# Long convolution and two mixture-of-experts layers: tokens packed without padding columns, and a new order of work in three places

## The chip, the cores and the metric

The kernel runs on one core of a Trainium2 chip. The metric is the time of one execution on the device in microseconds; the median of several executions counts.

## The reference, cut to what matters

```python
# attn: x, v [2, 11456, 128]; pos_emb [11456, 64]; w1 [64, 64]; w2 [64, 128]
h_filt = (np.maximum(pos_emb @ w1, 0.0) @ w2) * np.exp(-0.01 * pos)[:, None]
Uf = np.fft.rfft(x * v, n=2 * S, axis=1)
Hf = np.fft.rfft(h_filt, n=2 * S, axis=0)
x = x * np.fft.irfft(Uf * Hf[None], n=2 * S, axis=1)[:, :S, :]      # then [22912, 128]
# twice (the first time with modality_bias[modality_id] added to the logits):
logits = x @ w_gate                                   # 8 experts
e_idx = argmax(logits); gate_w = softmax(logits)[e_idx]
for e in range(8):
    out[mask] = gate_w[mask, None] * (np.maximum(x[mask] @ w1[e], 0.0) @ w2[e])   # w1 [128, 1024]
```

All matrices are fp32. A long causal convolution per channel is followed by two layers in which each token goes to one of eight experts.

## The kernel before, in words

There are four stages, each a block of its own with a barrier of all engines behind it: the convolution up to its inner inverse (`convolution`), the outer inverse with the first routing (`inverse_stage`), and two expert stages (`experts`, called with `then` for the first, which also routes for the second).

**Convolution.** The sequence is laid out as a two-dimensional transform: J = 91 columns (held as JP = 96) by 128 samples, 181 outer frequencies of which 92 are kept (K1), 128 inner ones. It begins with the filter. In 16 groups TensorE makes the hidden layer (`hidden`, L288), VectorE applies ReLU and window (L458) into one of two buffers `weighed`, TensorE makes four outputs of 2 x 128 columns (`output`, L295), and ScalarE copies the group with two activations, even and odd (L393), into `stage`. When all are copied ScalarE issues four stores of the filter's upper 64 channels to memory (`h_d`, L398); SP's signal loads (`load_signals`, L217) wait for these stores, since they go to the same slots. Then for each half of the channels (half 0, half 1):

- *Transform.* 24 chunks in the order `ORDER`: F chunks are of the filter, S chunks of signals (x times v). TensorE makes eight matmuls a chunk (L311) into one of two PSUM halves; ScalarE (L364 to L369) and VectorE (F chunks only, L425, L427) evict them into `A`. VectorE's `mix` multiplies x and v (L415) and folds them (L419), `LEAD[half]` chunks ahead of the chunk that uses them. LEAD is 2 in the first half and 3 in the second.
- *Spectral loop.* T = 46 steps. `forward(t)` on TensorE (L321, two matmuls of 384 columns), `filter_out(t)` on ScalarE (L376), `multiply(t)` on VectorE (L434, two operations), `combine(t)` on VectorE (L445, L447), `inverse(t)` on TensorE (L330, two of 256 columns), `back_out(t)` on ScalarE (L383), store by SP. TensorE's order is forward(t), inverse(t-2); VectorE's is multiply(t), combine(t-1). SP loads each step's matrices six steps ahead.

**Inverse stage.** TensorE begins with six warm-up matmuls on `inv`, for whose load it waits (L822). In 16 groups: `outer` (L793, 32 matmuls of 96 columns a half), ScalarE's copy (L929), VectorE's `mix` (L847 into `y`, L853 into `x1T`), `gate` (L808) on six chunks of 128 tokens a group, ScalarE's copies (L940, L943), VectorE's `choose` and `put`, which give each token its row among those of its expert (the last operations of a group are L887 and L888), and 12 scatters on POOL (L1000), one for each 128 tokens. Columns 91 to 95 are padding and are routed to nowhere. After group i's scatters POOL waits for those of group i - 1 in `settle`. VectorE ends the stage with `finish`, which copies the experts' end rows to `ends_i` (L666) and computes the table of tiles (up to L699); then SP writes a block of padding rows behind each expert (`Router.pad`, L709) and waits for them.

**Expert stages.** 49 tiles of 512 tokens in a software pipeline (`pipeline`); each engine runs its steps with a lag in tiles. L1162 to L1164 are the first layer, L1179 to L1181 the second, L1263 scales the results into `rows[s]` (four buffers), POOL scatters them (four a tile, L1381 or L1385). POOL's list of steps is `[(settle, 1), (scatter, 0)]`: before tile k it waits for the scatters of tile k - 1. ScalarE's scaling of tile k waits for `rows_free`, that is for settle(k - 4), in the first expert stage; in the second VectorE's `meta` does. The first expert stage ends with `finish` and `pad` as well. L1366 is POOL's first operation of an expert stage.

## Time and profile before

| | us |
|---|---|
| runs | 2048.15, 2060.18, 2061.36 |
| median | 2060.18 |
| profiled execution | 2052.0 |
| its span | 2050.2 |
| TensorE busy in the span | 1843.9 (90%) |
| VectorE, ScalarE, GpSimd busy | 1242.7, 1001.2, 583.7 |

Stages on the axis of the span: filter phase to 47.9, transforms and spectral loops to about 450, inverse stage to 752, first expert stage to 1424, second to 2050.2. A row of the timeline has the start, the duration, the engine, the line of the kernel, the operation with its tiles and shapes, how many instructions are merged, and in brackets how long the engine was idle before and what ended that. A fp32 matmul has two records. A queue's name (ACTq, SPq) marks the issue of a DMA, not the transfer.

### The profile page before, as it was taken

How to read it: one execution, taken by the hardware profiler on the slowest of the kernel's cores; microseconds unless marked ns; L12 is line 12 of the kernel's file. 1: busy time of each engine (PE TensorE's matmuls, PEld its weight loads, DVE VectorE, ACT ScalarE, POOL GpSimd, SP SyncE). 2: the span in 40 equal slices, each digit the busy share in tenths (PEclk: the TensorE clock that was granted, in tenths of full speed). 3: DMA queues.
4: the chain of work that ended last, by engine and by line, in shares of the span. 5: the costliest groups of instructions: out<-in, count | busy, mean ns of one | idle time of the engine just before them, and what ended most of it. 6: DMA issues, size and time to landing. Idle time of an engine off the chain costs nothing. (4 is left out here: it accounts for less than half of the span.)

```text
span 2050.2 us, 34634 instructions
## 1 busy us (share of the span) xinstructions
PE 1843.9 (90%) x9508; PEld 1547.3 (75%) x9508; DVE 1242.7 (61%) x3396; ACT 1001.2 (49%) x2185; POOL 583.7 (28%) x603
## 2 busy tenths in 40 slices
PE   8789988989989619999999999993999999999986
PEld 6665576559989517888888888893788888888886
DVE  1668776754767716777777777764555555555542
ACT  3563376432333305555555555551555555555543
POOL 0000000002777750333333333334033333333323
PEclk9899999987888759999999999996999999999998
DMA  4858694767999747777777777683666665665682
GB/s 142 218 140 254 202 235 141 214 186 216 323 301 319 241 155 272 239 250 255 250 253 252 247 252 254 242 326 119 245 232 207 225 234 207 225 234 207 229 308 110
DMA packets 193268, 469.51 MB, mean 229 GB/s; under 512 B 24691, under 2 KB 75455, under 8 KB 192792
## 3 DMA queue, kind: packets, MB, share of 16 engines
q1 hardware_dynamic: 163288, 412.13, 61.2%
q0 software_dynamic: 18688, 35.99, 4.9%
q10 hardware_dynamic: 11200, 20.26, 2.9%
q8 instruction: 45, 0.74, 0.2%
q14 instruction: 47, 0.39, 0.1%
HBM read 366.14 MB, written 105.28 MB: 230 GB/s over the span
## 5 line engine op out<-in xcount | busy, mean ns | idle before, releaser
L1306 DVE SCALAR_TENSOR_TENSOR m_hid<-m_pH,m_hid 128x512 fp32r<-128x512 f32 x784 | 540.9, 690 | 449.8 <-ACT m_hid L1241 443.9
L1241 ACT ACTIVATE m_hid<-m_pH 128x512 fp32r<-128x512 f32 x784 | 470.5, 600 | 534.4 <-PE m_pH L1164 534.4
L1162 PE MATMUL m_pH<-m_xT,m_w 128*128 128x512 f32 (+1 forms) x864 | 347.5, 402 | 7.8 <-DMA m_w<-halves 5.2
L1179 PE MATMUL m_pO<-m_hid,m_w 128*128 128x512 f32 (+1 forms) x864 | 323.0, 374 | 10.3 <-issue 10.3
L1381 POOL DMA_INDIRECT rows<-m_rows,m_idx x196 | 190.5, 972 | 476.9 <-ACT m_rows L1263 415.0
L1164 PE MATMUL m_pH<-m_xT,m_w 128*128 128x512 f32 (+1 forms) x864 | 323.3, 374 | 0.0
L1163 PE MATMUL m_pH<-m_xT,m_w 128*128 128x512 f32 (+1 forms) x864 | 322.5, 373 | 0.0
L1181 PE MATMUL m_pO<-m_hid,m_w 128*128 128x512 f32 (+1 forms) x864 | 321.5, 372 | 0.0
L1180 PE MATMUL m_pO<-m_hid,m_w 128*128 128x512 f32 (+1 forms) x864 | 320.3, 371 | 0.0
L1385 POOL DMA_INDIRECT out_dram<-m_rows,m_token x196 | 190.4, 972 | 429.8 <-ACT m_rows L1263 367.9
L1000 POOL DMA_INDIRECT rows<-oi_rows,oi_idx x192 | 196.4, 1023 | 102.0 <-issue 92.7
L1179 PEld LDWEIGHTS m_pO<-m_hid,m_w 128*128 128x128 f32 x864 | 163.9, 190 | 40.0 <-issue 11.5
L1162 PEld LDWEIGHTS m_pH<-m_xT,m_w 128*128 128x128 f32 x864 | 164.9, 191 | 28.6 <-DMA m_w<-halves 5.9
L1164 PEld LDWEIGHTS m_pH<-m_xT,m_w 128*128 128x128 f32 x864 | 164.0, 190 | 29.6
L1181 PEld LDWEIGHTS m_pO<-m_hid,m_w 128*128 128x128 f32 x864 | 163.8, 190 | 29.6
L1180 PEld LDWEIGHTS m_pO<-m_hid,m_w 128*128 128x128 f32 x864 | 164.0, 190 | 28.9
L1163 PEld LDWEIGHTS m_pH<-m_xT,m_w 128*128 128x128 f32 x864 | 165.1, 191 | 18.9
L311 PE MATMUL conv_pA<-conv_W,conv_stage 96*128 96x184 f32 x768 | 133.9, 334 | 30.1 <-DVE conv_stage L419 14.7
L434 DVE TENSOR_TENSOR conv_stage<-conv_pA,conv_stage 128x512 f32<-128x512 f32 x184 | 118.6, 687 | 62.8 <-ACT conv_stage L376 62.7
L311 PEld LDWEIGHTS conv_pA<-conv_W,conv_stage 96*128 96x128 f32 x768 | 125.9, 198 | 38.4 <-DVE conv_stage L419 16.1
L793 PE MATMUL oi_pY<-oi_inv,oi_C 91*128 91x96 f32 x1024 | 142.7, 308 | 0.8 <-DVE oi_y L847 0.8
L793 PEld LDWEIGHTS oi_pY<-oi_inv,oi_C 91*128 91x128 f32 x1024 | 141.6, 224 | 1.3 <-issue 1.2
(192 smaller groups left out, 2303.1 us busy)
## 6 DMA issues: line engine op xcount, KB each, us to landing
m_w<-halves SPq DMA_DIRECT2D x216, 1024.0 KB, 7.2
conv_stage<-in_inner_dram SPq DMA_DIRECT2D x92, 256.0 KB, 3.1
inner_back<-conv_stage SPq DMA_DIRECT2D x92, 256.0 KB, 3.1
oi_C<-inner_back SPq DMA_DIRECT2D x32, 728.0 KB
m_x<-rows SPq DMA_DIRECT2D x88, 264.0 KB, 2.7
halves<-m_parts SPq DMA_DIRECT2D x33, 512.0 KB, 9.5
halves<-oi_parts ACTq DMA_DIRECT2D x32, 512.0 KB
conv_stage<-in_x_dram SPq DMA_DIRECT2D x32, 384.0 KB, 6.9
```

The source lines that it names most:

```text
L311: last = nc.tensor.matmul(pA[:, n % 2, d // 2, d % 2 * 2 * K1:(d % 2 + 1) * 2 * K1], of(slot(half, n))[:, d].rearrange("p e s -> p (e s)") ...
L793: last = nc.tensor.matmul(pY[:, half, eo, t * JP:(t + 1) * JP], C[:, i % 2, half, eo, t, part * 128:(part + 1) * 128], inv[:, ((0, 1), (2, ...
L1000: pool.indirect_dma_start(rows_d, bass.IndirectOffsetOnAxis(r.idx[:, s, t:t + 1], 0), rows[:, s, t, :], None, bounds_check=E * CAP + TILE ...
L1162: nc.tensor.matmul(out, high, xT[:, s % 2, 0, cols], start=True, stop=False, skip_group_check=skip)
L1163: nc.tensor.matmul(out, high, xT[:, s % 2, 1, cols], start=False, stop=False, skip_group_check=skip)
L1164: last = nc.tensor.matmul(out, low, xT[:, s % 2, 0, cols], start=False, stop=True, skip_group_check=skip)
L1179: nc.tensor.matmul(out, high, hid[:, s % 2, c, 0, cols], start=(c == 0 and t == 0), stop=False, skip_group_check=skip)
L1180: nc.tensor.matmul(out, high, hid[:, s % 2, c, 1, cols], start=False, stop=False, skip_group_check=skip)
L1181: last = nc.tensor.matmul(out, low, hid[:, s % 2, c, 0, cols], start=False, stop=(c == FC - 1), skip_group_check=skip)
L1241: nc.scalar.activation(hid[:, s % 2, c, 0, 0:TILE], pH[:, c % HB, 0:TILE], ACT.Relu).then_inc(H_high, 1)
L1306: nc.vector.scalar_tensor_tensor(hid[:, s % 2, c, 1, 0:TILE], pH[:, c % HB, 0:TILE], 0.0, hid[:, s % 2, c, 0, 0:TILE].bitcast(F32), ALU.ma ...
L1381: pool.indirect_dma_start(next_rows, bass.IndirectOffsetOnAxis(r.idx[:, s, t:t + 1], 0), rows[:, s, t, LEAD:LEAD + ROW], None, bounds_chec ...
```

## The change

- Convolution: `output` is split by halves. The first pass, beside `hidden`, makes the upper 64 channels only (four matmuls of 128 columns a group), a second pass the lower 64; `weighed` keeps all 16 groups; one activation copies a group's half. The four stores of the upper channels are issued by SP once the first pass is copied, ahead of its signal loads. LEAD is (3, 3). VectorE's loop is multiply(t), combine(t).
- Inverse stage: the padding columns are left out, 91 columns a matmul instead of 96, so 91 chunks instead of 96: a group has five or six (`FIRST`), and 10 or 12 scatters. `x1T` holds all groups, the sums are written straight into it, `y` is gone. Five warm-up matmuls of 384 columns on `consts`, ahead of the wait for `inv`.
- Routing: `ends_i` is copied within the last `put`; `finish` has two operations fewer; its scratch lies in `xT`'s room; `pad` is split, experts 0, 2, 4, 6 and the spare block on SP, the others on ScalarE's queue.
- Expert stages: POOL's list is `[(settle, 2), (scatter, 0)]`.

```diff
-WARM = 6
+WARM = 5
-    LEAD = (2, 3)
+    LEAD = (3, 3)
...
@@ convolution, SP
             sp.dma_start(W[:, :], outer_d).then_inc(W_in, 16)
+            sp.wait_ge(h_copied, GROUPS)
+            for i in range(4):
+                at = CHUNKS_H + 2 * i
+                sp.dma_start(h_d[:, 2 * i * CD * ST:2 * (i + 1) * CD * ST],
+                             stage[0:JP, at:at + 2].rearrange("p c w -> p (c w)")).then_inc(h_stored[i], 16)
...
@@ convolution, TensorE
-            def output(i):
+            def output(half, i):
+                turn = (1 - half) * GROUPS + i
                 pe.wait_ge(win_done, i + 1)
-                if i >= 2:
-                    pe.wait_ge(h_copied, 2 * (i - 1))
+                if turn >= 4:
+                    pe.wait_ge(h_copied, turn - 3)
                 for t in range(GRP):
-                    last = nc.tensor.matmul(pA[0:JP, 1, i % 2 * 2 + t // 2, t % 2 * 2 * D:(t % 2 + 1) * 2 * D],
-                                            weighed[:, i % 2, t * JP:(t + 1) * JP], w2s, start=True, stop=True)
+                    last = nc.tensor.matmul(pA[0:JP, 1, turn % 4, t * 2 * HD:(t + 1) * 2 * HD],
+                                            weighed[:, i, t * JP:(t + 1) * JP],
+                                            w2s.rearrange("p (e d) -> p e d", e=2)[:, :, half * HD:(half + 1) * HD],
+                                            start=True, stop=True)
...
                 if i >= 2:
-                    output(i - 2)
+                    output(1, i - 2)
+            for i in range(GROUPS):
+                output(0, i)
...
@@ convolution, ScalarE
-            for i in range(GROUPS):
-                act.wait_ge(h_ready, i + 1)
-                for eo in range(2):
-                    src = pA[0:JP, 1, i % 2 * 2:i % 2 * 2 + 2].rearrange("p b (t e d) -> p e d b t", t=2, e=2)
-                    nc.scalar.activation(h[:, :, eo, i * GRP:(i + 1) * GRP].rearrange("p d (b t) -> p d b t", t=2),
-                                         src[:, eo], ACT.Copy).then_inc(h_copied, 1)
-            act.wait_ge(h_copied, 2 * GROUPS)
-            for i in range(4):
-                at = CHUNKS_H + 2 * i
-                act.dma_start(h_d[:, 2 * i * CD * ST:2 * (i + 1) * CD * ST],
-                              stage[0:JP, at:at + 2].rearrange("p c w -> p (c w)")).then_inc(h_stored[i], 16)
+            for turn in range(2 * GROUPS):
+                half, i = 1 - turn // GROUPS, turn % GROUPS
+                act.wait_ge(h_ready, turn + 1)
+                nc.scalar.activation(
+                    h[:, half * HD:(half + 1) * HD, :, i * GRP:(i + 1) * GRP].rearrange("p d e t -> p e d t"),
+                    pA[0:JP, 1, turn % 4].rearrange("p (t e d) -> p e d t", t=GRP, e=2), ACT.Copy
+                    ).then_inc(h_copied, 1)
...
@@ convolution, VectorE
-                for t in range(T + 1):
-                    if t < T:
-                        multiply(half, t)
-                    if t >= 1:
-                        combine(half, t - 1)
+                for t in range(T):
+                    multiply(half, t)
+                    combine(half, t)
...
@@ Router
         def partitions():
             c = chain(6)
             c.done()
+            if isinstance(k, int) and k == self.last:
+                v.tensor_copy(self.ends_i[:, :], self.carry[:, :]).then_inc(self.ended, 1)
...
-        c.link(v.tensor_copy(self.ends_i[:, :], self.carry[:, :]))
-        dve.sem_inc(self.ended, 1)
-        c.link(v.tensor_tensor(count, self.carry[:, :], self.base[:, :], ALU.subtract))
-        c.link(v.tensor_scalar(self.count_i[:, :], count, float(HALF - 1), None, ALU.add))
+        c.link(v.scalar_tensor_tensor(self.count_i[:, :], self.carry[:, :], float(HALF - 1), self.base[:, :],
+                                      ALU.add, ALU.subtract))
...
+    def pad(self, queue, which, rows_d):
+        queue.wait_ge(self.made, 3)
+        if which == 0:
+            queue.dma_start(rows_d[E * CAP:E * CAP + TILE].rearrange("(p s) w -> p s w", s=SUB),
+                            self.fill[:, :, :]).then_inc(self.emptied[which], 16)
+        queue.wait_ge(self.ended, 1)
+        for e in range(which, E, 2):
+            row = queue.value_load(self.ends_i[0:1, e:e + 1], min_val=0, max_val=E * CAP)
+            queue.dma_start(rows_d[bass.ds(row, TILE)].rearrange("(p s) w -> p s w", s=SUB),
+                            self.fill[:, :, :]).then_inc(self.emptied[which], 16)
+        queue.wait_ge(self.emptied[which], 16 * (E // 2 + 1 - which))
...
@@ inverse_stage
+GJ = GRP * J
+FIRST = [2 * GJ * i // 128 for i in range(GROUPS + 1)]
...
-            pe.wait_ge(inv_in, 16)
...
-                for cc in range(CC):
-                    k = i * CC + cc
+                for k in range(FIRST[i], FIRST[i + 1]):
...
             for _ in range(WARM):
-                nc.tensor.matmul(pG[0:JP, 0, 0:3 * JP], inv[:, 0, :], inv[:, :, :].rearrange("k m j -> k (m j)"),
-                                 start=True, stop=True, skip_group_check=True)
+                nc.tensor.matmul(pG[:, 0, 0:3 * 128], consts[:, 0:128], consts[:, :], start=True, stop=True,
+                                 skip_group_check=True)
+            pe.wait_ge(inv_in, 16)
...
             def mix(i, half):
                 dve.wait_ge(odd_copied, 2 * i + half + 1)
-                if i >= 1:
-                    dve.wait_ge(x1_done, 2 * (i - 1) + half + 1)
+                both = x1T[:, half, i * 2 * GJ:(i + 1) * 2 * GJ]
                 for m, op in enumerate((ALU.subtract, ALU.add)):
-                    nc.vector.tensor_tensor(y[:, half, m], pY[:, half, 0, 0:GC], odd[:, half], op).then_inc(y_done, 1)
+                    nc.vector.tensor_tensor(both[:, m * GJ:(m + 1) * GJ], pY[:, half, 0, 0:GJ], odd[:, half], op
+                                            ).then_inc(y_done, 1)
...
-                for t in range(n):
+                for t in range(B * chunks(i)):
...
@@ experts, POOL
-            pipeline(pool, TILES, 4, [(settle, 1), (scatter, 0)], BIG)
+            pipeline(pool, TILES, 4, [(settle, 2), (scatter, 0)], BIG)
```

## Rows read from the trace of the kernel before

**Rows 1.** The page: busy tenths in 40 slices; granted clock in tenths
```profile
PE   8789988989989619999999999993999999999986
...
PEclk9899999987888759999999999996999999999998
```

**Rows 2.** Timeline, filter phase: start, duration, engine, line, operation, count, idle before
```profile
15.35 1.89 PE L295 MATMUL conv_pA<-conv_A 128*96 128x256 f32 x8
...
17.72 1.89 PE L295 MATMUL conv_pA<-conv_A 128*96 128x256 f32 x8
```

**Rows 3.** Timeline, first signals of the convolution
```profile
47.92 4.80 ACTq L398 DMA_DIRECT2D filter_rows<-conv_stage  x4
...
65.95 1.22 DVE L415 TENSOR_TENSOR conv_stage<-conv_stage 96x1024 f32<-96x1024 f32 x1 [7.12 <-DMA conv_stage<-in_v_dram]
...
67.21 1.29 DVE L419 TENSOR_TENSOR conv_stage<-conv_stage 96x512 f32<-96x512 f32 x2
...
68.55 11.05 PE L311 MATMUL conv_pA<-conv_W,conv_stage 96*128 96x184 f32 x48 [9.03 <-DVE conv_stage L419]
...
80.05 2.76 PE L311 MATMUL conv_pA<-conv_W,conv_stage 96*128 96x184 f32 x16 [0.45 <-ACT conv_A L369]
```

**Rows 4.** Windows: stretch, busy of each engine, granted clock, share, GB/s
```profile
65.00:70.00 5.00, 1.45 (x5) 1.45 (x6) 3.98 (x5) 0.00 (x0) 0.00 (x0) 0.50 1.00 227
```

**Rows 5.** Timeline, spectral loop of the first half
```profile
202.03 1.29 DVE L434 TENSOR_TENSOR conv_stage<-conv_pA,conv_stage 128x512 f32<-128x512 f32 x2 [0.77 <-ACT conv_stage L376]
...
203.56 0.42 DVE L447 TENSOR_TENSOR conv_stage<-conv_stage 128x256 f32<-128x256 f32 x1
...
204.04 1.13 PE L330 MATMUL conv_pA<-conv_stage 128*128 128x256 f32 x4 [0.31 <-DVE conv_stage L447]
...
205.01 1.45 PE L321 MATMUL conv_pA<-conv_A,conv_stage 128*128 128x384 f32 x4
...
206.91 1.29 DVE L434 TENSOR_TENSOR conv_stage<-conv_pA,conv_stage 128x512 f32<-128x512 f32 x2 [0.77 <-ACT conv_stage L376]
```

**Rows 6.** Timeline of the inverse stage, with one stretch of the windows
```profile
454.07 6.07 PE L822 MATMUL oi_pG<-oi_inv 91*96 91x288 f32 x12 [6.28 <-DMA oi_inv<-in_outer_inv_dram]
...
486.14 3.73 PE L793 MATMUL oi_pY<-oi_inv,oi_C 91*128 91x96 f32 x32
...
513.42 0.97 POOL L1000 DMA_INDIRECT rows<-oi_rows,oi_idx  x1 [2.77 <-DVEq L890]
...
630.00:650.00 20.00, 19.13 (x122) 18.67 (x121) 14.23 (x46) 6.63 (x29) 15.35 (x16) 0.74 0.99 346
...
710.85 0.11 DVE L888 CAST oi_rows<-numbers 128x12 uint32<-128x12 f32 x1
...
750.63 0.97 POOL L1000 DMA_INDIRECT rows<-oi_rows,oi_idx  x1 [0.30 <-issue]
```

**Rows 7.** Timeline, end of the first expert stage
```profile
1390.64 0.97 POOL L1381 DMA_INDIRECT rows<-m_rows,m_idx  x1 [8.03 <-DVEq L1347]
...
1418.25 0.21 DVE L699 SCALAR_TENSOR_TENSOR tiles<-m_tv 128x54 int32<-128x54 f32 x1
...
1419.29 0.97 POOL L1381 DMA_INDIRECT rows<-m_rows,m_idx  x1 [2.63 <-issue]
...
1426.22 1.86 POOL L1366 MEMSET m_rows<- 128x2112 f32 x1 [2.13 <-POOLq L58]
```

**Rows 8.** Timeline, end of the kernel
```profile
2043.46 0.97 POOL L1385 DMA_INDIRECT out_dram<-m_rows,m_token  x1 [2.08 <-DMA out_dram<-m_rows,m_token]
```

**Rows 9.** Timeline, transform of both halves up to their first forward matmul
```profile
138.72 5.83 PE L321 MATMUL conv_pA<-conv_A,conv_stage 128*128 128x384 f32 x12 [3.08 <-ACT conv_A L369]
...
281.04 7.75 PE L311 MATMUL conv_pA<-conv_W,conv_stage 96*128 96x184 f32 x48 [2.08 <-DMA conv_stage<-filter_rows]
...
333.00 2.85 PE L321 MATMUL conv_pA<-conv_A,conv_stage 128*128 128x384 f32 x8 [3.08 <-ACT conv_A L369]
```

**Rows 10.** Windows, fullest stretch of a spectral loop
```profile
165.00:185.00 20.00, 18.76 (x66) 11.93 (x67) 16.01 (x33) 7.91 (x17) 0.00 (x0) 1.00 0.96 290
```

117 lines of the change are left out of this document (59 added, 58 removed).

## The prediction

> **What bounds it now.** I read the page's slices first: TensorE is busy eight or nine tenths almost everywhere, with holes where the stages meet, and the clock line is below full in the second slice, at those borders and through slices 9 to 15 [rows 1]. So the change can only pay where TensorE waits or where another engine ends a stage. Four places follow from the timeline.
>
> First, the start of the convolution. The filter phase runs in periods of 2.37 us [rows 2]: one 384-column matmul and four of 256 columns, so 1408 columns at 1.683 ns each. TensorE sets that pace. Then the filter's upper rows are stored from ScalarE's queue at 47.92, the signals may only be loaded behind them, VectorE gets the first pair at 65.95 and TensorE stands still for 9.03 us ahead of 68.55 [rows 3]. The clock is at its lower level there, 0.50 [rows 4].
>
> Second, the spectral loops (46 steps, twice). Two steps take 206.91 - 202.03 = 4.88 us, 2.44 each, with no engine full: TensorE waits 0.31 for VectorE's combine, VectorE 0.77 for ScalarE's copy [rows 5]. It is a circle: combine, inverse matmul (204.04), the next forward (205.01), ScalarE's copy, multiply (206.91), combine again. It closes once in two steps, because combine(t-1) stands behind multiply(t).
>
> Third, the inverse stage: the last tokens have their places at 710.85, but POOL issues scatters until 750.63 without a pause [rows 6]. POOL ends that stage, not the pads nor VectorE. Fourth, the drain between the two expert stages: POOL waits 2.63 us for its own scatter ahead of the last tile [rows 7], and likewise ahead of the three before it, and once at the kernel's end [rows 8].
>
> **The parts.** (a) Filter halves. Matmul columns stay the same: 16 x (384 + 4 x 128) and then 16 x 4 x 128. By 1.683 ns the first pass has periods of 1.51 us. The third output started at 15.35, the first thus two periods earlier, 10.6; the sixteenth upper output ends near 10.6 + 15 x 1.51 + 0.6 = 34 us, and its copy at 34.5. The lower pass takes 16 x 0.86 = 13.8 us and ends near 47.6, where the old phase ended; ScalarE's 32 copies keep their number and size and hide in it. What is not shown is a 128-column matmul with 96-column weights. The nearest row is the inverse stage's 96 columns with 128-column weights: 32 records in 3.73 us, 0.117 at most and 0.112 without the last one's drain, where their columns alone would be 0.081 [rows 6, 2]; against 0.108 for 128 columns that is at worst 256 records x 0.004 to 0.009 = 1 to 2 us. Below nothing it can't be, as the columns remain. I take 0. The Trainium skill (TensorE: Matmul & The Clock Gate, LDWEIGHTS) has the load as columns over 1.2 GHz, an estimate of 80 ns for 96 columns, so hidden: by it the term is 0 as well and the upper end falls away. The same rule has 107 ns for 128 columns, so cutting the inverse matmuls from 96 to 91 columns gives nothing, which the 0.112 already says.
>
> (b) The stores go to SP and start at 34.5 instead of 47.92; they are ahead of the signal loads on the same queue, as they must be by their semaphores, and ScalarE no longer spends 4.80 us issuing them [rows 3]. The first pair landed 18.0 us after the first store was issued; now that is 52.5, when TensorE is 4.6 us into its first two chunks, which need 2 x 2.6 us (48 records, three chunks, take 7.75 us at full clock [rows 9]). So the 9.03 us go. The three chunks behind the gap took 80.05 - 68.55 = 11.5 us at the low clock [rows 3] against 7.75: another 3.3 on their own 11.05. What is late next is VectorE: with the new lead the first mix (1.22 + 1.29 us) goes in front of the third filter chunk's eviction, and the fourth chunk behind waits for that: 2.5 us back. Net 12.3 - 2.5 = 9.8; I take 10, bounds 0 (signals land 10 us later than reckoned) and 12.3.
>
> (c) Lead 3 in the first half. From the chunk at 80.05 to the first forward matmul at 138.72 it takes 58.7 us; the second half, which has lead 3 already, takes 333.00 - 281.04 = 52.0 for the same chunks, with its own loads competing [rows 3, 9]. Term 6.7; bounds 0 and 8.
>
> (d) Combine(t) directly behind multiply(t). The circle now closes over three steps: 4.9 + 0.04 over 3 = 1.65 us, no longer the limit. 0.04 is the gap of one VectorE operation that waits for the last (65.95 + 1.22 to 67.21 [rows 3]). VectorE's own step is 1.29 + 0.04 + two combines of 0.42 that overlap a little: 2.1. TensorE's: 2 x 384 + 2 x 256 columns x 1.683 = 2.15. TensorE becomes the bound: 0.29 x 92 = 26.7 us. Each loop also fills and drains about 1 us sooner, which I leave for the range. The transfers: a step loads and stores 0.52 MB, 244 GB/s at 2.15 us; the fullest stretch moved 290 GB/s at a share of 0.96 with TensorE no less busy than elsewhere [rows 10]. Six matrices are loaded ahead, so I take no wait. Bounds 13 (half of it given back) and 31.
>
> (e) Inverse stage, packed. 91 chunks instead of 96, so 182 scatters, not 192; the other engines' work shrinks a little, off the path. From 513.42 (group 1) to 750.63 POOL made 179 steps of 1.325 us [rows 6]. Eight of the ten dropped scatters lie behind 513.42: 10.6 us. Group 0 has five chunks, and the warm-up begins at the barrier (near 452, with data that is there) instead of 454.07: ten records of 384 columns at the low clock, 0.64 each, end about 1 us earlier. So 1.5 more; term 12. The chain ahead of POOL keeps 14.1 us a group (513.4 to 710.85, 14 groups) against POOL's 11.4 x 1.33 = 15.1, so POOL remains behind and the bound; if it caught up, the end could still not be later than the chain makes it, about 726 (710.85 and twelve scatters), before POOL's own. Bounds 3 and 15. The split pads and the early copy of the ends finish at least 25 us before POOL here: 0, under cover of POOL; without that cover the SP queue's eight pads would cost what (f) says.
>
> (f) First expert stage's drain. POOL's five last tiles start at 1390.64; without the waits twenty scatters of 1.28 (0.97 + 0.30) put the last at 1414.9 instead of 1423.12 (1419.29 and three more) and the next stage, 3.1 us later as before, at 1418.0. But VectorE's table ends at 1418.46 [rows 7]. It gets about 0.5 earlier by two instructions less, 0.4 later since the last tile's scaling now waits for a buffer that POOL frees one scatter later. The pads, four and five to a queue, are issued in some 6 us even at the 1.2 us of one store in [rows 3], from near 1409, and are done before that. With the barrier I put the next stage at 1419.0 instead of 1426.22: 7.2; bounds 4 and 8.2. In the steady tiles the later settle costs nothing: POOL has long issued its scatter, then waits over 8 us for the next tile (1390.64's row), and frees the buffer in that time. (g) The last wait at the end goes: 2.08 - 0.30 = 1.8 [rows 8].
>
> **Sum.** 10 + 6.7 + 26.7 + 12 + 7.2 + 1.8 = 64.4 us off the profiled execution's 2052.0: 1987.6. Fill and drain of the loops would give 2 to 4 more. The median of the runs is 2060.18, 8 above the profiled one, the lowest 2048.15. I predict 1986.
>
> **Rivals.** *Transfers take the loops* (0.12): matrices come late beside the filter rows and signals, half of (d) is lost: 2000. For it: share 0.96 already; against: that stretch lost no TensorE time. *Signals late or the groups starved* (0.10): (b) and most of (e) go: 2006. *The reordering does nothing* (0.04), since another wait closes the loops at 2.44, and (b) fails as well: 64 - 27 - 10 = 27 left, 2025; with (c) and part of (e) gone too it is within 1%. *The clock* (0.03): two fuller loops are granted less. At a mean clock c they take 196/c; at 0.74, seen in the inverse stage with TensorE as busy as 19.13 of 20 us [rows 6], they cost 70 us more and eat everything; from 0.69 down the kernel is slower by over 1%, about 2082. Against it: the loops run at 1.00 now with 18.76 of 20 us busy [rows 10], and the experts at full with no gap. The Trainium skill (TensorE: Matmul & The Clock Gate, the HAM clock gate) says the throttle is the idle state and that the current limit needs three busy cores of a die; by that rule this rival's price is 0, and the 0.50 in the gap [rows 4] agrees with its first half.
>
> **Numbers.** Chances: as forecast 0.71, the others as given. The range takes the first three cases and the terms' bounds, not all at once, and 8 us of scatter: 1966 to 2020. Apart by over 1% (what a measurement can tell): faster 0.93, within 0.04, slower 0.03.
>
> **What would show it.** Stores on SP near 34 us; no gap of 9 us near 60; forward matmuls starting near 122 instead of 138.72; multiply every 2.15 us with combine right behind; 182 scatters, the stage ending near 739 on the old time axis; POOL without 2 us waits in the drains. Wrong would be: a loop pitch above 2.3, a clock below 1 in the loops, POOL idle between groups, or VectorE waiting for signals.

## The result, and the profile after

The changed kernel takes 1983.14 us, the median of four runs (1980.43 to 1988.19), against 2058.3 (2048.15 to 2061.36) for the kernel before, of which a fourth run, 2056.41, has joined the three shown above: a ratio of 0.9646 with a 95% interval of 0.9607 to 0.9685. The forecast was 1986, range 1966 to 2020. The profiled execution took 1983.54 us, with a span of 1981.8; that of before had 2050.2, so 68.4 us lie between the two traces, and the forecast's sum was 64.4. The total hides errors of opposite sign, which a cut into stages shows. Each border is the start of one instruction, found in both timelines:

| stretch | before | after | gain | forecast |
|---|---|---|---|---|
| start to first forward matmul (a, b, c) | 138.72 | 122.78 | 15.9 | 16.7 |
| both spectral loops (d) | 228.9 | 205.2 | 23.7 | 26.7 |
| transform of the second half | 79.1 | 78.9 | 0.3 | 0 |
| last inverse matmuls to first scatter (e) | 43.7 | 36.8 | 6.9 | } 12 |
| first scatter to the first experts' memset (e) | 263.4 | 251.0 | 12.4 | } |
| first experts (f) | 672.4 | 666.9 | 5.5 | 7.2 |
| second experts, to the end (g) | 624.0 | 620.2 | 3.8 | 1.8 |

A loop is counted from its first forward matmul to the next half's first signal matmul, and, in the second half, to the inverse matmuls of its last step. Those start at 406.88 in the changed kernel. In the kernel before the last row of inverse matmuls holds eight records, of two steps, and the last step's start in its middle, at 446.77. TensorE in the kernel before, then in the changed one:

```profile
445.80 1.99 PE L330 MATMUL conv_pA<-conv_stage 128*128 128x256 f32 x8 [1.60 <-DVE conv_stage L447]
```
```profile
406.88 1.13 PE L338 MATMUL conv_pA<-conv_stage 128*128 128x256 f32 x4 [0.86 <-DVE conv_stage L453]
```

**The page.** The rows that answer to [rows 1]: the hole and the low clock in the second slice are gone; the weak slices where the expert stages begin and the clock below full from slice 9 on to the first of these are still there.

```profile
PE   8899999979898079999999999994999999999996
...
PEclk9999999989888589999999999996999999999998
```

**The start.** In the timeline of the changed kernel the upper rows are stored from SP's queue at 34.67 instead of 47.92, VectorE has its first pair at 55.76 instead of 65.95, TensorE's longest wait up to 75 is 1.65 us where [rows 3] have 9.03, and its first forward matmul starts at 122.78 instead of 138.72 [rows 9].

```profile
34.67 4.72 SPq L260 DMA_DIRECT2D filter_rows<-conv_stage  x4
...
64.63 5.25 PE L319 MATMUL conv_pA<-conv_W,conv_stage 96*128 96x184 f32 x32 [1.65 <-DVE conv_A L433]
...
122.78 6.96 PE L329 MATMUL conv_pA<-conv_A,conv_stage 128*128 128x384 f32 x12 [3.08 <-ACT conv_A L379]
```

**A loop.** The same loop as in [rows 5], now with combine right behind multiply (151.72, 153.04) and 2.15 us from multiply to multiply; TensorE's matmuls have no idle time ahead of them. But at 160.05 TensorE has waited 1.46 us for a matrix, and once more at 163.03, with the transfer engines at a share of 1.06 in that stretch (in the windows' row behind the granted clock).

```profile
151.72 1.29 DVE L440 TENSOR_TENSOR conv_stage<-conv_pA,conv_stage 128x512 f32<-128x512 f32 x2
...
153.04 0.42 DVE L451 TENSOR_TENSOR conv_stage<-conv_stage 128x256 f32<-128x256 f32 x1
...
153.88 1.29 DVE L440 TENSOR_TENSOR conv_stage<-conv_pA,conv_stage 128x512 f32<-128x512 f32 x2
...
160.05 1.56 PE L329 MATMUL conv_pA<-conv_A,conv_stage 128*128 128x384 f32 x4 [1.46 <-DMA conv_stage<-in_inner_dram]
```

The windows of the stretch around it:

```profile
158.00:166.00 8.00, 5.99 (x22) 3.70 (x21) 5.17 (x11) 2.62 (x6) 0.00 (x0) 1.00 1.06 332
```

The first steps of both loops do not have the full clock in this trace. It is 0.50 up to 128.5, so for 5.7 us of the first loop, and again from 306.0 to 309.4 in the second. The windows of the first ten microseconds of each loop:

```profile
122.78:132.78 10.00, 10.00 (x25) 6.18 (x26) 6.04 (x13) 2.13 (x5) 0.00 (x0) 0.71 0.09 21
305.63:315.63 10.00, 10.00 (x28) 6.10 (x29) 6.84 (x14) 2.73 (x6) 0.00 (x0) 0.83 0.17 52
```

**The inverse stage.** The warm-up starts at 412.29 and the first 64 outer matmuls take 7.69 us; before, 96-column ones took 13.81 from 459.94 on. From the second group's start (465.51) to the last scatter, issued at 691.42, POOL has no pause.

Timeline of the changed kernel, TensorE and POOL:

```profile
412.29 4.91 PE L828 MATMUL oi_pG<-consts 128*128 128x384 f32 x10 [4.28 <-PEq L58]
...
419.28 7.69 PE L800 MATMUL oi_pY<-oi_inv,oi_C 91*128 91x91 f32 x64 [2.08 <-DMA oi_C<-inner_back]
...
429.59 5.26 PE L814 MATMUL oi_pG<-gates,oi_x1T 128*128 128x144 f32 x20 [2.62 <-DVE oi_x1T L858]
...
443.67 1.12 POOL L1008 DMA_INDIRECT rows<-oi_rows,oi_idx  x1 [30.02 <-issue]
...
465.51 0.97 POOL L1008 DMA_INDIRECT rows<-oi_rows,oi_idx  x1 [5.92 <-DVEq L893]
...
691.42 0.97 POOL L1008 DMA_INDIRECT rows<-oi_rows,oi_idx  x1 [0.30 <-issue]
```

The windows show why, the changed kernel's first and then one of the kernel before. In the changed kernel the granted clock rises within the warm-up, and it is full under the outer matmuls; in the kernel before it is 0.50 from the warm-up on until past 480, for some 27 us, with TensorE busy but for one wait of 2.72.

```profile
414.00:416.00 2.00, 2.00 (x5) 1.06 (x5) 0.00 (x0) 0.38 (x2) 0.00 (x0) 0.69 0.60 148
420.00:422.00 2.00, 2.00 (x20) 2.00 (x19) 0.00 (x0) 0.00 (x0) 0.00 (x0) 1.00 1.05 255
```
```profile
470.00:472.00 2.00, 2.00 (x11) 2.00 (x11) 0.00 (x0) 0.00 (x0) 0.00 (x0) 0.50 0.83 268
```

**The drains.** The last five tiles of the first experts, in POOL's timeline, without the four waits of over 2 us; the pads go out on both queues at 1349.96; VectorE's table ends at 1359.33 and the next stage starts at 1361.60. From the first of these tiles to there it takes 28.93 us, where [rows 7] have 1426.22 - 1390.64 = 35.58. At the end of the kernel the last eight scatters follow each other at 0.30, so the 2.08 of [rows 8] are gone.

```profile
1332.67 0.97 POOL L1391 DMA_INDIRECT rows<-m_rows,m_idx  x1 [8.38 <-DVEq L1357]
...
1349.96 4.58 SPq L716 DMA_DIRECT2D rows<-m_fill  x4
...
1358.48 0.97 POOL L1391 DMA_INDIRECT rows<-m_rows,m_idx  x1 [0.30 <-issue]
...
1359.12 0.21 DVE L705 SCALAR_TENSOR_TENSOR tiles<-m_room 128x54 int32<-128x54 f32 x1
...
1361.60 1.86 POOL L1376 MEMSET m_rows<- 128x2112 f32 x1 [2.15 <-POOLq L58]
```

### The profile page after: what moved, and what is told of

Read it like the earlier page. It is cut to its first block and busy times, and to the rows that moved or that the text cites. A ratio compares the mean times of both kernels' runs of the same rounds, so it can differ in the third digit from the quotient of the medians.

```text
span 1981.8 us, 34785 instructions
## 1 busy us (share of the span) xinstructions
PE 1814.6 (92%) x9614; PEld 1540.7 (78%) x9614; DVE 1245.9 (63%) x3394; ACT 998.8 (50%) x2170; POOL 573.5 (29%) x594
## 5 line engine op out<-in xcount | busy, mean ns | idle before, releaser
L1187 PE MATMUL m_pO<-m_hid,m_w 128*128 128x512 f32 (+1 forms) x864 | 322.7, 374 | 10.2 <-issue 10.1
L1171 PE MATMUL m_pH<-m_xT,m_w 128*128 128x512 f32 (+1 forms) x864 | 321.9, 373 | 0.0
L1008 POOL DMA_INDIRECT rows<-oi_rows,oi_idx x182 | 184.9, 1016 | 93.8 <-issue 81.8
L329 PE MATMUL conv_pA<-conv_A,conv_stage 128*128 128x384 f32 x368 | 138.3, 501 | 8.2 <-ACT conv_A L379 6.2
L800 PE MATMUL oi_pY<-oi_inv,oi_C 91*128 91x91 f32 x1024 | 132.9, 294 | 2.9 <-DMA oi_C<-inner_back 2.1
```

The costliest lines, as they stand in the source:

```text
L1008: pool.indirect_dma_start(rows_d, bass.IndirectOffsetOnAxis(r.idx[:, s, t:t + 1], 0), rows[:, s, t, :], None, bounds_check=E * CAP + TILE ...
L1171: nc.tensor.matmul(out, high, xT[:, s % 2, 1, cols], start=False, stop=False, skip_group_check=skip)
L1187: nc.tensor.matmul(out, high, hid[:, s % 2, c, 0, cols], start=(c == 0 and t == 0), stop=False, skip_group_check=skip)
```

## The experiments

Twelve kernels were run in four groups, each group on one chip beside the kernel before. The chips differ, and one fact has to be known to read the ratios: the kernel before takes 2052.35 us on the chip of runs 5 to 8, and 2121.1, 2118.76 and 2121.36 on those of 1 to 4, 9 to 11 and 12. For the changed kernel the stretches below put the difference into the scatters and the first experts. So a ratio is held against the unchanged kernel of the same chip where there is one, and the stretches of the profile are compared where a part has its place. All stretches, in us, in the order of the table above (loops apart; e5 and e9 are the changed kernel as it is):

| run | start | loop 1 | transform | loop 2 | to first scatter | scatters | experts 1 | experts 2 |
|---|---|---|---|---|---|---|---|---|
| before | 138.7 | 115.1 | 79.1 | 113.8 | 43.7 | 263.4 | 672.4 | 624.0 |
| after | 122.8 | 104.0 | 78.9 | 101.2 | 36.8 | 251.0 | 666.9 | 620.2 |
| e1 | 123.2 | 115.4 | 79.7 | 115.1 | 36.1 | 321.0 | 680.4 | 619.7 |
| e2 | 130.1 | 102.5 | 81.3 | 102.3 | 35.3 | 305.9 | 681.7 | 619.3 |
| e3 | 132.2 | 101.3 | 78.0 | 102.1 | 35.5 | 323.2 | 684.1 | 622.8 |
| e4 | 123.3 | 103.1 | 81.8 | 102.0 | 42.8 | 317.6 | 676.4 | 621.9 |
| e5 | 123.9 | 102.3 | 80.7 | 100.2 | 42.5 | 253.2 | 667.7 | 618.6 |
| e6 | 122.8 | 103.0 | 81.1 | 102.2 | 42.1 | 252.4 | 667.9 | 622.2 |
| e7 | 123.4 | 102.7 | 78.7 | 100.2 | 41.0 | 256.2 | 677.0 | 620.1 |
| e8 | 123.4 | 104.1 | 82.4 | 101.0 | 37.3 | 260.7 | 666.7 | 620.8 |
| e9 | 123.1 | 101.6 | 78.9 | 101.2 | 34.5 | 320.6 | 682.1 | 620.4 |
| e10 | 123.1 | 101.4 | 80.3 | 102.3 | 34.5 | 312.5 | 683.6 | 624.2 |
| e11 | 123.5 | 101.5 | 78.4 | 100.2 | 35.8 | 321.9 | 687.9 | 620.2 |
| e12 | 139.2 | 101.4 | 79.6 | 100.2 | 43.8 | 328.0 | 680.5 | 624.0 |

### e1: combine late again

```diff
-                for t in range(T):
-                    multiply(half, t)
-                    combine(half, t)
+                for t in range(T + 1):
+                    if t < T:
+                        multiply(half, t)
+                    if t >= 1:
+                        combine(half, t - 1)
```

> The changed kernel with only the order of VectorE's loop put back: combine(t-1) behind multiply(t). Theory (the circle of three engines sets 2.44 us a step): two steps take 4.88 us again, and with two loops of 45 intervals (0.29 x 90 = 26.1) and the 2.6 us back that the changed kernel loses at 158 to 165, the profiled span is 22 to 26 us over 1981.8. Rival (TensorE was never held by this circle, the pitch came down through the earlier stores or the lead): the pitch stays near 2.15, the time within 5 us.

Measured: ratio 0.9893 (0.9861 to 0.9926); the changed kernel itself has 0.9745 on another chip with nearly the same time for the kernel before (e9). The steps alternate between 2.73 and 2.15 us, 4.88 for two, as in [rows 5]; the two loops take 230.6 us, where e2, e3 and e4 on that chip have 204.7, 203.4 and 205.1. That is 25.5 to 27.2 us for the place of one call in the loop. The expected total of 1981.8 plus 22 to 26 was missed (the span is 2090.7), since this chip is another one: its scatter stretch alone is 321.0.

VectorE's multiplies in e1's timeline:

```profile
149.90 1.29 DVE L440 TENSOR_TENSOR conv_stage<-conv_pA,conv_stage 128x512 f32<-128x512 f32 x2 [0.20 <-ACT conv_stage L386]
...
152.63 1.29 DVE L440 TENSOR_TENSOR conv_stage<-conv_pA,conv_stage 128x512 f32<-128x512 f32 x2 [0.77 <-ACT conv_stage L386]
...
154.79 1.29 DVE L440 TENSOR_TENSOR conv_stage<-conv_pA,conv_stage 128x512 f32<-128x512 f32 x2 [0.20 <-ACT conv_stage L386]
```

### e2: lead two again in the first half

```diff
-    LEAD = (3, 3)
+    LEAD = (2, 3)
```

> The changed kernel with the first half's lead back at two chunks. Theory (c): the first forward matmul moves from 122.78 to about 129.5, 6.7 us later, all of it on the path: span near 1988.5. Rival (the 16 us at the start all come from the stores, the lead is hidden): 0 to 2 us.

Measured: ratio 0.9749 (0.9717 to 0.9777). The first forward matmul comes at 130.10; in the five runs on this chip and e9's that leave lead and stores as changed (e1, e4, e9 to e11) it is 123.06 to 123.45, 123.23 in the mean. So the lead is worth 6.9 us where it stands. In the total it can't be seen: the scatter stretch differs by more between executions on this chip (305.9 here, 317.6 to 323.2 in its neighbours).

TensorE in e2's timeline:

```profile
130.10 6.83 PE L329 MATMUL conv_pA<-conv_A,conv_stage 128*128 128x384 f32 x12 [3.08 <-ACT conv_A L379]
```

### e3: the stores wait for the whole filter

```diff
-            sp.wait_ge(h_copied, GROUPS)
+            sp.wait_ge(h_copied, 2 * GROUPS)
```

> The changed kernel in which SP waits for all 32 copies of the filter before it stores the upper rows, as the kernel before did from ScalarE's queue. Theory (b): the stores go near 48.6 instead of 34.67, TensorE stands about 9 us ahead of its first signals and works at the lower clock behind: first forward matmul 10 us later (12.3 at most), span near 1992. Rival (the lead and VectorE's work behind would absorb it): under 4 us.

Measured: ratio 0.9781 (0.9749 to 0.9814). The stores go out at 47.57 instead of 34.67, VectorE waits 9.31 us for its first pair, which it has at 63.97 instead of 55.76, and the first forward matmul starts at 132.20, 8.9 us later than the 123.3 of e4. Theory (b) holds with 9 for the expected 10.

e3's timeline:

```profile
47.57 4.71 SPq L260 DMA_DIRECT2D filter_rows<-conv_stage  x4
...
132.20 5.83 PE L329 MATMUL conv_pA<-conv_A,conv_stage 128*128 128x384 f32 x12 [3.08 <-ACT conv_A L379]
```

### e4 and e6: which part of the new warm-up counts

e4 puts the warm-up of the kernel before back; e6 keeps the new one's time and columns and takes away rows alone:

```diff
-            for _ in range(WARM):
-                nc.tensor.matmul(pG[:, 0, 0:3 * 128], consts[:, 0:128], consts[:, :], start=True, stop=True,
-                                 skip_group_check=True)
-            pe.wait_ge(inv_in, 16)
+            pe.wait_ge(inv_in, 16)
+            for _ in range(6):
+                nc.tensor.matmul(pG[0:JP, 0, 0:3 * JP], inv[:, 0, :], inv[:, :, :].rearrange("k m j -> k (m j)"),
+                                 start=True, stop=True, skip_group_check=True)
```

```diff
-                nc.tensor.matmul(pG[:, 0, 0:3 * 128], consts[:, 0:128], consts[:, :], start=True, stop=True,
+                nc.tensor.matmul(pG[:, 0, 0:3 * 128], consts[0:91, 0:128], consts[0:91, :], start=True, stop=True,
```

> The changed kernel with the inverse stage's warm-up as before: six matmuls of 288 columns over 91 rows, behind the load of their operand. Theory (the new warm-up raises the clock before the first outer matmuls, the old one never did): the clock stays at 0.50 through the first 64 outer matmuls, they take about 13.8 us instead of 7.69, the first scatter comes 6 to 7 us later, span near 1988. Rival, the prediction's own reading (the warm-up is only shorter): 1 to 2 us.

> The changed kernel with its warm-up cut from 128 to 91 rows of the same operands: the same ten records of 384 columns at the same time, at the barrier. Theory (what raised the clock was the 128 rows): it stays at 0.50 through the 64 outer matmuls, which take 13 to 14 us, and the first scatter comes 6 to 7 us later than in the unchanged kernel. Rival (the early start or the 384 columns did it): as in the unchanged kernel, 64 outer matmuls in 7.7 us, no difference.

Measured: e4 0.9752 (0.9717 to 0.9787), e6 0.9714 (0.9673 to 0.9754), where the unchanged kernel beside e6 has 0.9677 (0.9645 to 0.971). In both the 64 outer matmuls take 13.8 to 13.9 us, and the first scatter comes 42.8 and 42.1 us after the last inverse matmuls. In e6 the clock is 0.50 in every two-microsecond stretch from the warm-up to 441, as it was in the kernel before.

The outer matmuls in e4's timeline, then in e6's, and one of e6's windows under them:

```profile
423.48 13.80 PE L800 MATMUL oi_pY<-oi_inv,oi_C 91*128 91x91 f32 x64
```
```profile
421.27 13.93 PE L800 MATMUL oi_pY<-oi_inv,oi_C 91*128 91x91 f32 x64
```
```profile
425.00:427.00 2.00, 2.00 (x11) 2.00 (x11) 0.00 (x0) 0.00 (x0) 0.00 (x0) 0.50 1.03 351
```

### e5: the changed kernel again

> The changed kernel as it is, on the chip of the next three runs. If its chip grants TensorE what the first one did, near 1983 with POOL without a pause in the inverse stage; if it grants less there, as in the four runs before (slices of 0.6 and 0.7 where the first had 0.8), POOL waits for placed tokens between groups, the stage is 30 to 50 us longer and the whole near 2045. In both cases the first forward matmul comes at 122.8 to 123.3 and each loop takes 101 to 104 us.

Measured: 1988.43 us, ratio 0.9677 (0.9645 to 0.971), no pause of POOL from the second group on. This run was to be the base for three others, and it gave the finding of the study. Its warm-up is the same to the instruction. By the clock in the two-microsecond stretches, it rose 2.9 us behind the warm-up's start in the first trace (0.69 from 414 to 416) and 5.1 us behind it here (0.86 from 417 to 419); it was full for 3.4 us and fell again under the outer matmuls, which took 13.01 us. The first scatter came 42.5 us after the last inverse matmuls, not 36.8.

The outer matmuls in e5's timeline, and the windows of the rise and of the fall:

```profile
419.93 13.01 PE L800 MATMUL oi_pY<-oi_inv,oi_C 91*128 91x91 f32 x64 [1.50 <-DMA oi_C<-inner_back]
```
```profile
417.00:419.00 2.00, 1.43 (x4) 0.53 (x2) 0.00 (x0) 0.00 (x0) 0.00 (x0) 0.86 0.97 248
421.00:423.00 2.00, 2.00 (x12) 2.00 (x11) 0.00 (x0) 0.00 (x0) 0.00 (x0) 0.50 1.05 244
```

Over all traces: where the warm-up has 91 rows (before, e4, e6, e12) the 64 outer matmuls took 13.80 to 13.93 us each time. Where it has 128 rows and five matmuls they were done in 7.35 to 7.90 us in seven traces (after, e1, e2, e3, e8, e9, e11) and in 12.5 and 13.0 in two (e5, e7). So the 6 us are real, but the changed kernel does not get them every time. Both of these are among the four in which the clock rose late, 5.1 to 5.5 us behind the warm-up's start. But a late rise alone does not lose them: it was as late in e1 and e11, whose ten warm-up records took 6.06 and 6.02 us.

### e7: settle one tile behind again

```diff
-            pipeline(pool, TILES, 4, [(settle, 2), (scatter, 0)], BIG)
+            pipeline(pool, TILES, 4, [(settle, 1), (scatter, 0)], BIG)
```

> The changed kernel with POOL settling a tile one behind again in both expert stages. Theory (f, g): four waits of 2.2 to 2.6 us come back in the drain of the first stage, less 2 us or so that data gave anyway: from the first tail tile's scatter to the next stage's memset 35.6 us as before instead of 28.9, so 6.6 more, and 1.8 more at the end: 8.4 us on the span. Rival (the shorter drain came from the split pads or the earlier copy of the ends): under 2 us.

Measured: ratio 0.9713 (0.9677 to 0.9749) beside 0.9677. The waits of 2.2 to 2.3 us are back, and one has become 3.87, right behind the pads that both queues issue from 1360.6 on: 36.81 us from 1342.45 to the memset at 1379.26, against 29.04 in e5, so 7.8. The first scatter of the kernel's last tile waits 2.09 again, and the stretch from the last eight scatters on is 13.65 against 11.87, 1.8 as expected.

POOL in e7's timeline:

```profile
1342.45 0.97 POOL L1391 DMA_INDIRECT rows<-m_rows,m_idx  x1 [8.17 <-DVEq L1357]
...
1365.37 0.97 POOL L1391 DMA_INDIRECT rows<-m_rows,m_idx  x1 [3.87 <-issue]
...
1379.26 1.86 POOL L1376 MEMSET m_rows<- 128x2112 f32 x1 [2.14 <-POOLq L58]
```

### e8: ten scatters more

The ten columns that packing left empty are scattered too (their indices point nowhere; their rows are zeroed first):

```diff
-                for t in range(B * chunks(i)):
+                for t in range(n):
```

> The changed kernel with twelve scatters in every group again, 192 instead of 182; the ten more hold no tokens (their indices point nowhere). Theory (e) where POOL ends the inverse stage without a pause: 8 of the ten lie behind the second group's start, so the stage ends 10.6 us later. Rival (the matmuls and VectorE's placing set the groups' pace, as where the clock is lower): each more fits into POOL's pause ahead of the next group, 0 to 3 us. The unchanged kernel of this call says by POOL's pauses which of the two holds on this chip.

Measured: ratio 0.9728 (0.9696 to 0.9759) beside 0.9677, 9.4 us by the medians. The stretch from the first scatter on is 260.7 us against 251.0, 253.2, 252.4 and 256.2 in the four traces with 182 scatters and no pauses, 7.5 above their mean. Where the rest went shows when the stretch is cut at the second group's start. Up to there it takes 21.85 us, against 21.84 to 23.3 in the four: POOL waits for the second group in any case, 3.10 us here and 5.92 in the first trace, and the two more scatters of the first group cost nothing. Behind it, up to the memset, it takes 238.88 us against 229.16 to 232.90. These also differ in how many single scatters took longer than 0.97 us; without those excesses (7.1 us here, 7.6 to 11.2 there) it is 231.8 against 221.6 to 221.8, and 231.8 in the kernel before as well. So eight scatters are worth 10.1 us, eight steps of 1.28, where 10.6 was expected. POOL ends the stage on that chip, and packing is worth its scatters.

POOL in e8's timeline, the second group's start:

```profile
470.12 0.97 POOL L1008 DMA_INDIRECT rows<-oi_rows,oi_idx  x1 [3.10 <-DVEq L893]
```

### e9, e10: the changed kernel on a third chip, and an attempt to beat it

e10 makes three additions:

```diff
-WARM = 5
+WARM = 8
...
-                    if half == 0 and t == 2 * R + 3:
+                    if half == 0 and t == 5 * R + 3:
                         load_signals(1, 0)
...
             outer(0, 1)
+            for _ in range(4):
+                nc.tensor.matmul(pG[:, 0, 0:3 * 128], consts[:, 0:128], consts[:, :], start=True, stop=True,
+                                 skip_group_check=True)
             gate(0)
```

> The changed kernel as it is, beside the next two on one chip. Of its ten runs of the inverse stage's start so far (with variants that leave that start alone) the first scatter came 35.3 to 37.3 us after the convolution's last inverse matmuls in five and 41.0 and 42.5 in two; here one or the other, and the loop of the first half loses 1 to 2.6 us near 160.

> The changed kernel with three additions: the first signals of the second half are loaded at step 33 instead of 15; the inverse stage's warm-up has eight matmuls instead of five, so that it reaches to the arrival of the first operands; four more of them fill TensorE's 2.6 us wait ahead of the first gate matmuls. Theory (the loss near 160 is transfers that meet; whether the clock is full under the first outer matmuls is chance in the changed kernel and would be certain here): no step of the first loop over 2.3 us behind the first three, 1 to 2.6 us gained; the outer and gate matmuls at full clock, first scatter 33 to 35 us after the last inverse matmuls, 2 to 8 us gained; in all 3 to 10 us less than the unchanged kernel of this call. Rival for the warm-up (91-row matmuls let the clock fall whatever ran ahead of them): it falls near 421 again, the four fillers cost 5 us at the low clock, first scatter 40 us or more and the time up to 3 us longer.

Measured: e9 0.9745 (0.9717 to 0.9774), e10 0.9733 (0.9705 to 0.9761), which can't be told apart. The late load only moved the stall: the first loop has a step of 2.82 us at 199.38 instead of one of 2.96 at 160.88, and takes 101.4 against 101.6. The warm-up did what it was for. In e10 the clock rose 4.2 us behind the start, past 416, and yet the outer matmuls took 7.28 us, the gate matmuls behind the fillers had the full clock, and the first scatter came 34.5 us after the last inverse matmuls. But e9 had an early rise and 34.5 too, so this pair shows no gain; and as the shorter warm-up kept the clock in seven traces of nine, one trace of the longer one does not show that it protects. On this chip POOL pauses ahead of most groups, so it does not end the stage, and a sooner start need not be kept.

TensorE in e10's timeline, and one of POOL's pauses ahead of a group in e9's timeline:

```profile
419.82 7.28 PE L800 MATMUL oi_pY<-oi_inv,oi_C 91*128 91x91 f32 x64
```
```profile
622.04 0.97 POOL L1008 DMA_INDIRECT rows<-oi_rows,oi_idx  x1 [2.76 <-DVEq L893]
```

e9 shows another thing that the first trace does not have. In the drain of the first experts three engines stand at the same time: ScalarE for 5.69 us up to 1414.91, TensorE for 3.52 up to 1415.65, VectorE for 4.53 up to 1416.37; POOL then waits 5.19 for its third tile, and the drain takes 35.8 us instead of 29. POOL's second and third tile of the drain are 10.0 us apart there, and 10.5 to 12.4 in e2, e3, e10 and e11, all on two chips; in e1 and e4, on one of them too, it is 7.0 and 5.3, and in the first trace, e5, e6 and e8 5.4 to 5.7.

POOL in e9's timeline:

```profile
1421.94 0.97 POOL L1391 DMA_INDIRECT rows<-m_rows,m_idx  x1 [5.19 <-DVEq L1357]
```

### e11: the old pads

All pads on SP, and the ends copied behind the last placing:

```diff
-        for e in range(which, E, 2):
+        for e in range(E):
...
-            r.pad(act, 1, rows_d)
...
-            if isinstance(k, int) and k == self.last:
-                v.tensor_copy(self.ends_i[:, :], self.carry[:, :]).then_inc(self.ended, 1)
...
+        c.link(v.tensor_copy(self.ends_i[:, :], self.carry[:, :]))
+        dve.sem_inc(self.ended, 1)
```

> The changed kernel with all pads on SP's queue in every stage, and the ends copied where the table begins, behind the last placing. Theory (both are covered: by POOL's scatters in the inverse stage, by POOL and the table in the drain of the first expert stage): 0 to 1 us there, the drain from the first tail tile's scatter to the next memset 29.0 to 30. Rival (the drain got shorter by the pads): 3 to 7 us longer, as 8 pads take 8.02 us to issue where four on each queue take 4.6.

Measured: ratio 0.9754 (0.9728 to 0.978) beside e9's 0.9745, within the intervals; but in the drain the rival holds. POOL's last scatter is issued at 1439.59 and the table ends at 1441.84, yet the memset comes at 1449.07: SP's eight pads take 11.62 us from 1434.33 and end last. From the first tail tile to the memset it takes 40.37 us against 35.76 in e9 and 37.02 in e10, so 3.4 to 4.6 us for pads and copy together. In the kernel before SP issued the eight in 8.02 us under cover of POOL. SP in the timeline of before, then SP, POOL and VectorE in e11's:

```profile
1410.19 8.02 SPq L709 DMA_DIRECT2D rows<-m_fill  x8
```
```profile
1434.33 11.62 SPq L716 DMA_DIRECT2D rows<-m_fill  x8
...
1439.59 1.10 POOL L1388 DMA_INDIRECT rows<-m_rows,m_idx  x1 [0.30 <-issue]
...
1441.63 0.21 DVE L705 SCALAR_TENSOR_TENSOR tiles<-m_room 128x54 int32<-128x54 f32 x1
...
1449.07 1.86 POOL L1373 MEMSET m_rows<- 128x2112 f32 x1 [8.38 <-POOLq L58]
```

### e12: the kernel before with combine early, and nothing else

The edit is e1's, the other way round, in the kernel before.

> The kernel before with one edit alone: combine(t) directly behind multiply(t) in both loops. Theory (d): both loops go from 2.44 to 2.15 us a step, first forward to the second half's first signals 103 to 104 us instead of 115.1, and again 101 to 102 instead of 112.8 in the second; 22 to 25 us off the whole, as the putting back of the same lines cost 24.6 in the two loops of the changed kernel. The ratio to the kernel before is then 0.988 to 0.990 on any of the three chips seen. Rival (gains of the parts overlap, the loops come down only together with the earlier stores and the lead): ratio 0.995 or more.

Measured: ratio 0.9867 (0.9842 to 0.9892), slightly more than expected: 27.5 us of 2121.36. The loops take 101.4 and 100.2 us instead of 115.1 and 113.8, together 27.4 less. The rival is refuted: this part needs no other.

TensorE in e12's timeline, the first forward matmul and the second half's first signals:

```profile
139.25 2.85 PE L321 MATMUL conv_pA<-conv_A,conv_stage 128*128 128x384 f32 x8 [3.08 <-ACT conv_A L369]
...
240.64 2.73 PE L311 MATMUL conv_pA<-conv_W,conv_stage 96*128 96x184 f32 x16 [0.16 <-DVE conv_stage L434]
```

## Why the prediction was right, and where its steps were not

The order of the loops, the start and the dropped scatters came out by the mechanisms named and carry most of the gain. That the sum of 64.4 came within 4 us of the 68.4 measured is in part luck: (e) gave 7.3 more than its term, (d) and (f) gave 3.0 and 1.7 less.

**(a) to (c), the start: right.** 16.7 forecast, 15.9 measured. The undoings give 8.9 us for the stores (e3; 10 forecast) and 6.9 for the lead (e2; 6.7), and these add up to the whole, so the split of the filter cost nothing that can be seen. The stores were issued at 34.67, forecast near 34. VectorE had its first pair at 55.76, 3.3 us later than the 52.5 reckoned, which did no harm: four filter chunks stand ahead of the first signal chunk, and that one started at 60.25 with 1.34 us of waiting.

**(d), the loops: the mechanism right, the size right alone.** TensorE became the bound at 2.15 us a step exactly, and alone the order is worth 27.4 (e12; 26.7 forecast), 13.6 of it in the second loop, where the clock is full in both kernels. In the changed kernel's first trace 23.7 are left. Two things make up the 3.7 between them. One is the stall at 160: the prediction took "no wait", with six matrices loaded ahead, but between steps 12 and 18 two filter loads and a pair of signal loads are added to the stream at a share of 1.06. It costs 1.73 and 0.83 us over the pitch in the first trace, and 0.7 to 2.5 in the others with the short step, 1.9 of them in e12; so it explains 0.6 of the 3.7. That is the rival on the transfers at a fifth of its size (2.6 of 13). At 2.44 us a step no such stall is seen (the kernel before, e1).

The other is the clock over a loop's first steps, which the prediction did not ask about: e12 has 1.00 through both loops, the first trace 0.50 for 5.7 and for 3.4 us of them. The second loop, which has no stall, shows the price. It takes 100.2 us in the four traces whose clock is full throughout (e5, e7, e11, e12), 101.0 to 101.3 in the three with 0.50 for 3.4 us at its start (the first trace, e8, e9), and 102.0 to 102.3 in the five with 0.50 for 6.8 us around it (e2, e3, e4, e6, e10). So 1.1 us are lost in the first trace's second loop, and 2.0 is what is left for its first. TensorE waits the same 3.08 us ahead of the loop in all of them; why the clock falls there in some and not in others is open.

The window of e5's second loop, to be held against 305.63:315.63 of the first trace:

```profile
306.86:316.86 10.00, 9.40 (x33) 6.12 (x34) 7.86 (x17) 3.12 (x7) 0.00 (x0) 1.00 0.25 73
```

**(e), the inverse stage: the step that failed.** 12 forecast, with bounds of 3 and 15; 19.3 measured, outside them. Of that, 11.2 lie behind the second group's start, where the forecast had 10.6 for eight scatters; e8 gives 10.1 for eight by undoing, so the term is right. The other 8.0 lie ahead of it, where the forecast had 1.5: 6.9 ahead of the first scatter and 1.2 between it and the second group. The sentence that failed is that the ten warm-up records at the low clock "end about 1 us earlier". The warm-up was priced as work to be got through, and what it does to the clock behind it was not asked, though the trace of before had the answer to look for: the outer matmuls at 13.81 us for 64, twice the 0.112 that the prediction itself used for the same instruction at full clock. Behind the start of the last inverse matmuls the warm-up came 1.9 us sooner; the outer matmuls began 1.1 later behind it, the gate matmuls 6.2 sooner behind those, and 0.1 was lost from there to the first scatter: 6.9. Where the clock fell back, in e5, the stage's two stretches sum to 295.75 against 307.05: 11.3, near the forecast, which had left the clock out. The reading that POOL ends the stage holds on the first chip and that of e5 to e8; on the other three it does not, since POOL pauses ahead of the groups there.

**(f), (g), the drains: right in the first trace, one cover misjudged.** The drain gave 6.65 of 7.2, with POOL and the table ending nearly together as forecast (the last scatter at 1358.48, the table's end at 1359.33). Undoing the settle cost 7.8 and 1.8 (e7). The first experts gained only 5.5, as their steady part was 1.2 longer in this trace (638.0 against 636.8), and the second's was 2.1 shorter (608.3 against 610.4); in the other traces these parts scatter from 637.6 to 647.6 and from 606.5 to 612.3, so nothing is read from that. The split of the pads was put at nothing for the inverse stage, where POOL covers it, and the prediction named what would uncover it: a shorter drain. That is what the later settle made, and there the split and the early copy of the ends together earn 3.4 to 4.6 us on e11's chip. For the first chip it was not run; there the table starts at 1350.4, SP would begin 1.0 us later, take 8.02, and the memset follow 3.1 later as in e11, at 1362.5 instead of 1361.60: an estimate of 0.9.

**The other rivals.** Signals were not late and no group starved on the first chip. "A clock below 1 in the loops" was named as a sign of being wrong, and it did occur, but over the first 5.7 and 3.4 us alone; behind them the clock stayed at 1.00, so the rival on the slower side, with 70 us, had no ground, and what the low clock did cost is 3 us. On e9's chip the change is worth less: 52.5 us, at 0.9745, instead of 75.2. The stretches say where: the loops and the start gain as much as elsewhere; the scatters take 306 to 323 us with the packed columns against 328.0 with the old ones (e12, another chip of that kind), and the drain of 35.76 in e9 is no shorter than e12's 35.5.

## What to carry to other kernels

A loop that runs over several engines at a pitch that none of them fills has a circle; write out which step's work each instruction waits for, and move the consumer next to its producer before anything else is made faster. When a wait is removed in a drain, price again everything that it covered: here the pads were free until the settle moved. And when a change touches a warm-up or a gap, read the granted clock of the instructions behind it, not only the time of the warm-up itself; a saving that hangs on the granted clock needs more than one trace.

## What the runs showed of the hardware

**Rows of the operands and the clock.** Warm-ups of 91 rows never raised the granted clock in four traces (6.1 to 6.7 us of warm-up and 13.8 to 13.9 us of outer matmuls at 0.50), one of them with the same columns at the same moment as the 128-row one. Warm-ups of 128 rows raised it in all ten traces that have one. The outer matmuls, also of 91 rows, kept a full clock for 7 to 8 us in eight of these, and lost it in e5 and e7, with TensorE busy. It does not follow that all 128 rows are needed: in the kernel before the transform's matmuls, of 96 rows and 184 columns, began at 68.55 at 0.50, and the clock was full from 75.2 on. What separates 91 rows from these 96 was not tested. The windows of the kernel before, ahead of that rise and behind it:

```profile
68.50:74.50 6.00, 5.95 (x19) 5.95 (x20) 5.87 (x7) 0.63 (x1) 0.00 (x0) 0.50 0.95 216
75.50:79.50 4.00, 4.00 (x26) 3.75 (x25) 2.51 (x3) 3.67 (x6) 0.00 (x0) 1.00 1.03 234
```

**When it rises is not fixed.** The same ten records took from 4.91 to 6.21 us in nine traces, as the clock rose 2.9 to 5.5 us behind their start. The Trainium skill (TensorE: Matmul & The Clock Gate, The HAM clock gate) says that the number of matmuls at the low clock varies from run to run of one kernel; the traces agree.

**Chips differ, most in one stage.** From 460 to 700 us the mean granted clock is 0.80 in the first trace and 0.69 in e9, and POOL issued 178 scatters there against 136. With it go pauses of single outer matmuls with nothing that the profile names behind them (23 of 0.2 to 0.5 us in that stretch of e9, none in the first trace), and the standstill of three engines in the drain. What causes these was not settled: no run tells apart a lower clock that stretches the chain from a stall that lowers the clock.

The window of the whole stretch in the first trace, then in e9's:

```profile
460.00:700.00 240.00, 170.84 (x1196) 163.56 (x1196) 153.41 (x502) 70.31 (x294) 177.55 (x178) 0.80 0.81 272
```
```profile
460.00:700.00 240.00, 191.33 (x1063) 180.97 (x1062) 121.49 (x390) 59.13 (x245) 137.10 (x136) 0.69 0.67 228
```
